# An HGRN scan with a gated MLP on one core: the first block of w_in is loaded, rounded and given its rest in two halves by channel, and three steps of VectorE's opening order are moved

## The reference

```python
def _attn_ref(x, f_logit, lower_bound):          # x, f_logit: (2, 6080, 256)
    sig = 1.0 / (1.0 + np.exp(-f_logit))
    f = lower_bound + (1.0 - lower_bound) * sig
    i = 1.0 - f
    for t in range(S):
        h = f[:, t] * h + i[:, t] * x[:, t]
        y[:, t] = h

def _moe_ref(x, w_in, w_out):                     # w_in (256, 2048), w_out (2048, 256)
    h = x @ w_in
    relu6 = np.clip(h + 3.0, 0.0, 6.0)
    return (h * relu6 / 6.0) @ w_out
```

## Time and profile before

| | |
|---|---|
| median of 3 runs | 990.0 us (989.41 to 990.23) |
| the profiled execution, its own time | 989.92 us |
| its span, first to last instruction | 987.9 us |
| PE, matmuls | 982.0 us busy, 99% of the span |
| DVE (VectorE) | 817.5 us, 83% |
| ACT (ScalarE) | 715.0 us, 72% |
| POOL (GpSimd) | 204.2 us, 21% |

### The profile page before, as it was taken

How to read it: one execution, slowest core, us unless ns; L and a number is a source line. 1 busy time by engine, 2 the same in 40 slices (tenths; PEclk the granted TensorE clock), 3 DMA queues, 4 the chain that set the end, 5 groups by cost and what they waited for, 6 DMA issues and landing times.

```text
span 987.9 us, 13020 instructions
## 1 busy us (share of the span) xinstructions
PE 982.0 (99%) x4372; PEld 817.9 (83%) x4372; DVE 817.5 (83%) x1186; ACT 715.0 (72%) x1215; POOL 204.2 (21%) x141
## 2 busy tenths in 40 slices
PE   8999999999999999999999999999999999999998
PEld 8988888888888888888888888888888888888887
DVE  7998987887888898888788788788878878886765
ACT  7777677777767767767777776776777777677665
POOL 2543132122104013111210401311121140131000
PEclk9999999999999999999999999999999999999999
DMA  7211001101102100110110210101011011001001
GB/s 245 86 59 65 22 22 43 64 23 42 65 1 64 43 22 24 53 52 22 43 65 1 65 43 22 52 35 43 22 43 65 4 61 43 1 1 43 1 0 43
DMA packets 17522, 42.38 MB, mean 43 GB/s; under 512 B 2480, under 2 KB 3760, under 8 KB 17456
## 3 DMA queue, kind: packets, MB, share of 16 engines
q1 hardware_dynamic: 17168, 41.42, 12.6%
q10 hardware_dynamic: 288, 0.13, 0.0%
HBM read 29.10 MB, written 12.45 MB: 42 GB/s over the span
## 4 chain that ended last, share of the span: by engine, by line
PE 98%; DMA 1%; DVE 0%; SPq 0%; ACT 0%; issue 0%; ACTq 0%
PE y_ps L1013 16%; PE y_ps L1014 16%; PE y_ps L1012 16%; PE x_ps L995 8%; PE x_ps L996 8%; PE x_ps L997 8%; PE v_ps L997 4%; PE v_ps L996 4%; PE v_ps L995 4%; PE z_ps L996 2%; PE z_ps L997 2%; PE z_ps L995 2%; PE x_ps L967 2%; PE y_ps L978 1%; PE y_ps L979 1%; PE y_ps L980 1%
## 5 line engine op out<-in xcount | busy, mean ns | idle before, releaser
L747 DVE TENSOR_TENSOR g_lo<-g,g_hi 128x512 fp32r<-128x512 f32 x352 | 273.4, 777 | 46.6 <-ACT g_hi L488 44.7
L1012 PE MATMUL y_ps<-g_hi,w_out_hi 128*128 128x512 f32 x704 | 273.9, 389 | 0.0
L1014 PE MATMUL y_ps<-g_hi,w_out_lo 128*128 128x512 f32 x704 | 273.9, 389 | 0.0
L1013 PE MATMUL y_ps<-g_lo,w_out_hi 128*128 128x512 f32 x704 | 273.9, 389 | 0.0
L488 ACT CAST g_hi<-g 128x512 fp32r<-128x512 f32 x352 | 210.0, 623 | 17.0 <-DVE g L742 16.7
L1012 PEld LDWEIGHTS y_ps<-g_hi,w_out_hi 128*128 128x128 f32 x704 | 132.2, 188 | 27.5
L1013 PEld LDWEIGHTS y_ps<-g_lo,w_out_hi 128*128 128x128 f32 x704 | 132.2, 188 | 27.4
L1014 PEld LDWEIGHTS y_ps<-g_hi,w_out_lo 128*128 128x128 f32 x704 | 132.2, 188 | 27.3
L479 ACT ACTIVATE g<-z_ps,half 128x512 f32<-128x512 f32 x88 | 60.8, 691 | 63.4 <-DVE z_ps L725 61.0
L479 ACT ACTIVATE g<-v_ps,half 128x512 f32<-128x512 f32 x88 | 60.7, 690 | 56.0 <-DVE v_ps L737 56.0
L731 DVE TENSOR_TENSOR h_sb<-v_ps,h_sb 128x512 f32<-128x512 f32 x88 | 60.9, 692 | 34.2 <-PE v_ps L997 32.9
(11 more groups left out here) (162 smaller groups left out, 1826.9 us busy)
## 6 DMA issues: line engine op xcount, KB each, us to landing
z_sb<-in_z SPq DMA_DIRECT2D x21, 512.0 KB, 3.6
x_sb<-in_x SPq DMA_DIRECT2D x21, 512.0 KB, 4.5
out_y<-y_sb SPq DMA_DIRECT2D x20, 512.0 KB, 3.1
w_out_raw<-in_w_out SPq DMA_DIRECT2D x8, 256.0 KB, 8.0
w_in_raw<-in_w_in SPq DMA_DIRECT2D x6, 256.0 KB, 6.6
z_sb<-in_z SPq DMA_DIRECT2D x2, 480.0 KB, 3.5
x_sb<-in_x SPq DMA_DIRECT2D x2, 480.0 KB, 4.6
out_y<-y_sb SPq DMA_DIRECT2D x3, 256.0 KB, 2.1
```

Source lines behind the costliest of these rows:

```text
L747: nc.vector.tensor_tensor(g_lo[:, u], g[:, u], g_hi[:, u].bitcast(F32), ALU.subtract).then_inc(g_lo_ready[u], 1)
L1012: nc.tensor.matmul(out, w_out_hi[:, f, at], g_hi[:, u], start=opens, stop=False)
L1013: nc.tensor.matmul(out, w_out_hi[:, f, at], g_lo[:, u], start=False, stop=False)
L1014: return nc.tensor.matmul(out, w_out_lo[:, f, at], g_hi[:, u], start=False, stop=closes)
```

## The change

Block 0 of w_in is no longer loaded whole. The channel half k = 0 of both its hidden blocks (512 B twice per partition) takes its place in SP's list, and half k = 1 comes behind block 1. Each half has a load, a cast, a rest and semaphores of its own, and TensorE waits for the half that it reads. ScalarE casts the second half behind block 1; VectorE makes its rest behind block 1's. `w4_hi_ready` counts from block 1 on. Two more steps are moved on VectorE: `head_rest_of_op(0)` comes ahead of `head_drive(0, 1)`, and `rest_of_w4(3)` comes behind gate(1) and the rest of g(0), where it came behind gate(0).

```diff
+            def load_first_w_in(k):
+                sp.dma_start(raw_of(one_block(0))[:, 0, k:4:2], w_in[:, pair(0), k]).then_inc(first_w_in_loaded[k], 16)
...
-            load_w_in(0)
+            load_first_w_in(0)
             sp.dma_start(z_sb[:, 1, at], z[0, :, 1, at]).then_inc(head_z_loaded[1], 16)
             sp.dma_start(x_sb[:, 1, at], x[0, :, 1, at]).then_inc(head_x_loaded[1], 16)
             load_w_in(1)
+            load_first_w_in(1)
             load_w_in(2)
...
             def make_s3(i):
...
-                for j in range(at.start, at.stop):
+                if i == 0:
+                    pool.wait_ge(first_w4_ready[0], 1)
+                    pool.wait_ge(first_w4_ready[1], 1)
+                for j in range(max(at.start, 1), at.stop):
                     pool.wait_ge(w4_ready[j], 1)
...
+            def round_first_w4(k):
+                act.wait_ge(first_w_in_loaded[k], 16)
+                nc.scalar.copy(w7_hi[:, 0, k:4:2], raw_of(one_block(0))[:, 0, k:4:2]).then_inc(first_w4_hi_ready[k], 1)
...
             head_gate(0, 0)
-            round_w4(0)
+            round_first_w4(0)
             head_round_op(0)
             head_sig(1)
             head_gate(0, 1)
             round_w4(1)
+            round_first_w4(1)
             round_w4(2)
...
             def rest_of_w4(j):
-                dve.wait_ge(w4_hi_ready, j + 1)
+                dve.wait_ge(w4_hi_ready, j)
...
+            def rest_of_first_w4(k):
+                dve.wait_ge(first_w4_hi_ready[k], 1)
+                nc.vector.tensor_tensor(w7_lo[:, 0, k:4:2], raw_of(one_block(0))[:, 0, k:4:2],
+                                        w7_hi[:, 0, k:4:2].bitcast(F32), ALU.subtract).then_inc(first_w4_ready[k], 1)
...
             head_scan(0, 0)
-            rest_of_w4(0)
+            rest_of_first_w4(0)
+            head_rest_of_op(0)
             head_drive(0, 1)
-            head_rest_of_op(0)
             head_scan(0, 1)
             rest_of_w4(1)
+            rest_of_first_w4(1)
             head_rest_of_op(1)
             rest_of_w4(2)
             for v in range(HEAD):
                 head_gate_h(v)
                 if v > 0:
                     head_rest_of_g(v - 1)
-                if v == 0:
+                if v == 1:
                     rest_of_w4(3)
...
                 if p == 0 and part == W_LO:
-                    pe.wait_ge(w4_ready[j], 1)
+                    pe.wait_ge(first_w4_ready[k] if j == 0 else w4_ready[j], 1)
+                elif p == 0 and j == 0:
+                    pe.wait_ge(first_w4_hi_ready[k], 1)
                 elif p == 0:
-                    pe.wait_ge(w4_hi_ready, j + 1)
+                    pe.wait_ge(w4_hi_ready, j)
```

More of the change, by code:

```diff
@@ L100, in build @@
         lb_loaded = sem("lb_loaded")
-        w_in_loaded = [sem(f"w_in_loaded{j}") for j in range(BLOCKS)]
+        first_w_in_loaded = [sem(f"first_w_in_loaded{k}") for k in range(K)]
+        w_in_loaded = [None] + [sem(f"w_in_loaded{j}") for j in range(1, BLOCKS)]
         w_out_loaded = [sem(f"w_out_loaded{j}") for j in range(BLOCKS)]
+        first_w4_hi_ready = [sem(f"first_w4_hi_ready{k}") for k in range(K)]
+        first_w4_ready = [sem(f"first_w4_ready{k}") for k in range(K)]
         w4_hi_ready = sem("w4_hi_ready")
-        w4_ready = [sem(f"w4_ready{j}") for j in range(BLOCKS)]
+        w4_ready = [None] + [sem(f"w4_ready{j}") for j in range(1, BLOCKS)]
         w_sums_ready = sem("w_sums_ready")
@@ L769, in sum_weights @@
                 if o == S1_T1:
-                    for j in range(at.start, at.stop):
+                    if i == 0:
+                        dve.wait_ge(first_w_in_loaded[0], 16)
+                        dve.wait_ge(first_w_in_loaded[1], 16)
+                    for j in range(max(at.start, 1), at.stop):
                         dve.wait_ge(w_in_loaded[j], 16)
```

## The result

The changed kernel takes 990.91 us (median of 22 runs, 990.34 to 992.43), the kernel before 989.81 (22 runs beside them, 989.41 to 990.49). The ratio is 1.0013, with a 95% interval of 1.0007 to 1.0019: a loss of 1.1 us, clear of the noise and inside the 0.2% that the prediction called "same". Two executions of the kernel before in the last round of experiments took 1092 and 1664 us, at a mean granted clock of 0.85 and 0.56, and are left out of every ratio; with them the median of their round is 0.03 us higher.

What follows compares the result with a forecast made beforehand. PE was taken as the bound, busy 969.25 of 969.26 us from 15.66 us on, with 1.7 us idle before. 989.92 + 0.15 (first clip) + 0.60 (head_up(6)) = 990.67, forecast as 990.7 us, range 989.4 to 991.4.

Steps and rivals of the forecast that it cites:

- same: Whole kernel: a time within 0.2% of the kernel before, 988.0 to 992.0 us; chance 0.93.
- +0.15: First clip: PE's matmuls on block 2 start at 10.48 instead of 10.33, so the clip moves to 12.33; +0.15 us.
- +0.60: head_up(6): waits for gate(2), delayed behind block 3's moved w_lo, and starts at 17.40 instead of 16.80; +0.60 us.
- The lock: DVE and POOL in the head: a two-SBUF-input DVE instruction and a POOL one don't overlap; the later waits; +0.60 us.
- the rival with DVE first: Head: POOL's third w_out_lo comes after block 3's w_lo, so -0.43 + 0.15, giving 989.7 us; chance 0.25.
- Block 2: Opening: block 2's cast moves from 9.52 to 9.81, PE's matmuls on it to 10.48, the first clip +0.15 us.
- the price of the small rows: Block 0's load: 512 B rows at 32 ns each against 92 ns for 2 KB, interpolated; +0.29 us per engine.
- the 0.29: Block 0's two half loads together cost 0.29 us more than one, moving block 2's cast from 9.52 to 9.81.
- The prediction's line through two other row sizes: DMA row price: line through 22 ns at 256 B and 163 ns at 3.8 KB, giving 32 ns at 512 B.
- No idle behind head_up(6), and the queues: After head_up(6): PE busy 969 us in one piece; DMA transfers already queued, so the extra load's issue costs nothing.
- The halves' own gain: Opening: the sooner first half shrinks PE's first two waits, 0.4 and 0.6 us; none of it reaches the end.
- The slow rival: Block 2's load: 512 B rows cost as much as 2 KB ones, +2.06 + 0.60, giving 992.7 us; chance 0.05.

Runs made afterwards that it cites:

- after_third: The changed kernel run a third time, nothing altered; median 990.58 us over 11 runs, ratio 1.0007 to the kernel before.
- split_again: Second run of the changed kernel with block 3's w_lo put back behind gate(0); median 989.87 us over 11 runs.
- after_fill2: The changed kernel plus 8 matmuls on zeros in front of head_up(6), in PE's wait for gate(2); median 990.52 us over 11 runs.
- after_again: The changed kernel run once more, nothing altered; median 990.40 us over 11 runs, ratio 1.0005; its profile fell on an execution of 991.77.
- split_only: The changed kernel with block 3's w_lo put back behind gate(0); median 989.93 us over 11 runs, ratio 0.9999 to the kernel before.

## Why the prediction was right

The forecast was 990.7 (989.4 to 991.4), by +0.15 and +0.60. Measured are 990.91 in the first 22 runs, 990.59 over all 44.

*The lock,* that is, DVE and POOL waiting for each other. Shown. Forecast and profile: g_lo(0) 0.84 and 0.80 us; w_lo 1.7 and 1.77; PE's wait for gate(2) 1.0 and 0.88; head_up(6) against the clip +0.60 and +0.56. POOL went ahead in all seven profiles with the move, so the rival with DVE first has nothing left. What I read from one other place in the trace of before, at 36.88, carried over to a place where no such pair had stood.

*Block 2.* The step that was off is the +0.15 at the first clip. The clip was forecast at 12.33 and came at 12.07, 0.11 ahead of the kernel before. Block 2's cast began at 8.96, not 9.81, and did not set the clip: w_out's first load did (cast at 11.03), the path that the prediction had at 11.16 + 1.06 = 12.22, just ahead of block 2's. Four of the nine profiles with split loads have the clip on that path (the changed kernel, after_third, split_again, after_fill2), none of the five with a whole load.

The cast was forecast 0.29 later. Over the nine profiles with split loads it began between 8.85 and 10.20, 9.38 in the mean; over the five with a whole load between 9.07 and 9.52, 9.26 in the mean. A shift of 0.12 beside a spread of 1.35 us (0.45 with the whole load) shows neither the sign nor the size of the term. The spread is what the prediction lacked.

Nor do the runs show the price of the small rows that the 0.29 was made of. One microsecond seems to. DMA from 3 to 4 us, of the changed kernel:

```profile
DMA packets 330, 0.23 MB, mean 227 GB/s; under 512 B 28, under 2 KB 330, under 8 KB 330
q1 hardware_dynamic: 330, 0.23, 105.2%
```

and of the kernel before:

```profile
DMA packets 169, 0.27 MB, mean 267 GB/s; under 512 B 25, under 2 KB 80, under 8 KB 169
q1 hardware_dynamic: 166, 0.27, 97.1%
```

That is 73 us of engine time per MB (16 x 1.052 / 0.23) against 58 (16 x 0.971 / 0.27). But from 1 to 8 us, which holds all rows of block 0, it is 57 for the changed kernel (1.68 MB at 85.4%) and 55 for the one before (1.64 MB at 80.1%); over the nine profiles with split loads 51 to 57, 54 in the mean, and over the five with a whole load 53 to 56, 55 in the mean. The Trainium skill, DMA: Bandwidth & Descriptors, Specifications, has 512 B at line rate. Over the seven microseconds the traces agree so far as they can: with the 512 B rows in them they show no more engine time per byte. The prediction's line through two other row sizes did not hold. Why block 2 lands so unevenly with the split, by the order of the loads or by their number, was not tried apart and stays open.

*No idle behind head_up(6), and the queues.* Right: PE waits for nothing after 17.25. The last matmul starts at 984.82 for 984.53, +0.29 where head_up(6) had +0.45; the 0.16 between are small differences in the matmuls' spacing that I can't name.

*The halves' own gain.* As forecast, both first waits went (PE's first real matmuls at 6.46 for 7.30) and nothing of it arrived: PE waits for blocks 1 and 2 instead.

*What I had not thought of* is the clock. The prediction noted a granted clock of 1.00 and left it there. In after_again a quicker start left PE idle later and longer in one piece, block 2 was late, and the clock went. A fall of the clock goes with ten of the thirteen executions above 991.1; that a late block 2 stands behind each is argued from that one profile. Of the first 22 executions 15 had a mean clock of 1.000, and their median is 990.61, +0.8 over before: the falls account for 0.3 of the +1.1.

*Luck.* The stall of 0.6 us was forecast for the right reason. That the median lies within 0.3 us of the sum is in part luck: the profile was 0.30 below 990.67, 0.26 of it at the first clip, and the falls of the clock, which the sum doesn't hold, raised the median by as much.

The slow rival (2 KB price for every row) is out: it wanted block 2's cast at 11.7.

## What to carry to other kernels

Before moving a VectorE instruction with two SBUF inputs, look at what GpSimd holds and what it has waiting there: an instruction that costs 0.68 us in a free slot cost 1.77 behind a GpSimd one, and the engine that paid was the one that needed the next instruction. Work brought forward in an opening that waits for loads only moves TensorE's idle time, and one long gap can be dearer than two short ones, if it takes the clock with it. And where the time of single executions begins to spread, repeat the run until a profile falls on a long one: the profile of 990.37 us explained 0.45 us of 1.1.

## What the runs showed of the hardware that was not expected

The granted clock fell to 0.50 for 3.3 us after PE had been idle for 1.49 us at 9.0 to 10.5 us (after_again), but stayed at 1.00 after 1.37 us idle at 9.5 to 10.9 (split_only). The Trainium skill, TensorE: Matmul & The Clock Gate, Part 1, says of the clock's rise at a kernel's start that its point varies from run to run. Two like gaps with two outcomes would fit a fall that varies likewise, but one profile of each doesn't show it.

When VectorE has two instructions in a row with two SBUF inputs, GpSimd's waiting one was let in between them in all eight places that were looked at: between the first g_lo and block 3's w_lo in seven profiles (at 14.86 us in the changed kernel's), and behind 36.88 in the earlier trace rows.
